# A fused scan and two feed-forward layers on one core: another order around the lead's last step, the first step and both passages, and 24 products that nobody reads

## The reference

```python
mag = np.sqrt(a_re * a_re + a_im * a_im)
scale = np.minimum(mag, 0.999) / (mag + 1e-06)
for t in range(S):                       # a = (a_re, a_im) * scale
    new_re = ar * S_re - ai * S_im
    new_im = ar * S_im + ai * S_re
    S_re, S_im = new_re + outer(k[t], v[t]), new_im
    y[t] = q[t] @ S_re
# layer 1, d_ff 1536
xn = x / sqrt(mean(x * x) + 1e-06) * rms_g
x = (silu(xn @ w_gate) * (xn @ w_val)) @ w_out
# layer 2, d_ff 2048
h = x @ w_in
out = (relu(h) + log1p(exp(-abs(h)))) @ w_out2
```

## Time and profile before

| | us |
|---|---|
| median of the runs shown | 1146.66 |
| the profiled execution, whole | 1146.07 |
| its span, first to last instruction | 1144.2 |
| PE busy in the span | 1065.6 (93%) |
| ACT, DVE, POOL busy | 723.9, 650.9, 251.7 |

### The profile page before, as it was taken

One profiled execution on the slowest core, in us unless ns is written; L12 is line 12 of the kernel. 1 busy time (PEld: TensorE's weight loads), 2 busy tenths in 40 slices (PEclk: granted clock), 3 DMA queues, 4 the chain that ended last, 5 costly groups with the idle time before them and its releaser, 6 DMA issues.

```text
span 1144.2 us, 16983 instructions
## 1 busy us (share of the span) xinstructions
PE 1065.6 (93%) x5474; PEld 910.4 (80%) x5474; DVE 650.9 (57%) x2170; ACT 723.9 (63%) x1327; POOL 251.7 (22%) x259
## 2 busy tenths in 40 slices
PE   0577789999999999999999999989999999999997
PEld 0577778888888888888888877878888888888886
DVE  6999888888888988888886110221222213122211
ACT  5687656667666656666674434476666666676664
POOL 2122100010000101000100125633333333333332
PEclk9999989999999999999999999999999999999999
DMA  5888743444533533454444137510101001010000
GB/s 133 193 196 191 163 97 90 94 112 104 133 90 91 127 90 91 98 137 94 110 95 118 33 64 188 132 60 1 56 1 36 20 1 55 0 55 0 28 1 29
DMA packets 54322, 97.37 MB, mean 85 GB/s; under 512 B 9057, under 2 KB 30433, under 8 KB 54241
## 3 DMA queue, kind: packets, MB, share of 16 engines
q1 hardware_dynamic: 33504, 63.34, 18.5%
q0 software_dynamic: 15552, 25.96, 14.0%
q10 hardware_dynamic: 5184, 7.08, 2.2%
HBM read 49.02 MB, written 9.50 MB: 51 GB/s over the span
## 4 chain that ended last, share of the span: by engine, by line
PE 51%; issue 25%; POOL 11%; DVE 9%; ACT 2%; DMA 1%; POOLq 0%; SPq 0%; DVEq 0%; ACTq 0%
PE gbank L1492 25%; PE ybank L1492 12%; POOL pl L534 10%; DVE prep L892 4%; PE xbank L1521 3%; PE sbank L1509 3%; PE xbank L1520 3%; PE xbank L1524 2%; PE xbank L1500 1%; DVE pk L892 1%; DVE prep L926 1%; DMA pl<-hid 1%; PE sbank L1532 1%; ACT prep L575 1%; DMA a_in<-in_a 1%
## 5 line engine op out<-in xcount | busy, mean ns | idle before, releaser
L1492 PE MATMUL gbank<-xh,slab 128*128 128x512 f32 x1296 | 406.5, 395 | 2.5 <-ACT xh L619 1.5
L1492 PE MATMUL ybank<-ph,slab 128*128 128x512 f32 x1008 | 314.6, 393 | 5.5 <-ACT ytile L667 2.6
L1492 PEld LDWEIGHTS gbank<-xh,slab 128*128 128x128 f32 x1296 | 242.2, 190 | 51.5 <-ACT xh L619 1.7
L1492 PE MATMUL gbank<-xl,slab 128*128 128x512 f32 x648 | 254.1, 392 | 0.0
L1492 PEld LDWEIGHTS ybank<-ph,slab 128*128 128x128 f32 x1008 | 186.2, 188 | 43.7 <-issue 7.1
L1492 PE MATMUL ybank<-pl,slab 128*128 128x512 f32 x504 | 196.3, 389 | 0.0
L534 POOL TENSOR_TENSOR pl<-hid,ph 128x512 fp32r<-128x512 f32 x96 | 125.7, 1309 | 265.6 <-ACT ph L827 265.6
L1366 DVE SCALAR_TENSOR_TENSOR hid<-gbank,hid 128x512 f32<-128x512 f32 x72 | 49.8, 692 | 213.2 <-ACT hid L818 213.2
L511 POOL DMA_DIRECT2D pl<-hid x72 | 61.3, 852 | 484.1 <-ACT pl L660 476.2
L1492 PEld LDWEIGHTS gbank<-xl,slab 128*128 128x128 f32 x648 | 122.5, 189 | 26.4
L1492 PEld LDWEIGHTS ybank<-pl,slab 128*128 128x128 f32 x504 | 94.6, 188 | 20.1
(11 more groups left out here) (154 smaller groups left out, 1575.4 us busy)
## 6 DMA issues: line engine op xcount, KB each, us to landing
pl<-hid POOLq DMA_DIRECT2D x72, 256.0 KB, 3.7
mm<-pk SPq DMA_DIRECT2D x96, 144.6 KB, 3.2
a_in<-in_a SPq DMA_DIRECT2D x24, 384.0 KB, 3.7
kq_in<-in_kq SPq DMA_DIRECT2D x24, 384.0 KB, 3.4
ytile<-in_w ACTq DMA_DIRECT2D x36, 192.0 KB, 4.1
slab<-in_w POOLq DMA_DIRECT2D x36, 192.0 KB, 5.4
prep<-in_w SPq DMA_DIRECT2D x32, 192.0 KB, 2.6
v_in<-in_v SPq DMA_DIRECT2D x24, 192.0 KB, 3.5
```

What stands on the lines that cost most here:

```text
L1492: last = pe.matmul(out, slab[:, slot + part, cols], x, start=f, stop=l)
```

## The change

**TensorE.** In the lead's last step (m = 4) it also makes 24 products of 128x384 from the first weight block into `ybank[0]`, which nobody reads: 14 ahead of the turned keys of half 0, 4 behind the scores of half 0, 6 behind those of half 1. In the first step the value product of block 2 goes behind the outputs of half 0, the gate product of block 3 is drawn into it, between the scores of half 1 and `xt_of`. In the one step that has an x and no m (tile 4, i = 3), `xt_of` goes ahead of the output block. The small product on `okmin` goes behind the first tile of layer 2.

**ScalarE.** In the lead the copy of y's half 0 goes ahead of `mid_w2`. In the first step the copy of half 0 and `silu(0, 0)` come first, then `mid_w2`, then the copy of half 1; `x_sums` goes behind the second activation table load. In tile 4, i = 3, `xh_of` goes ahead of `hi`. `w2_hi_of` of the last slot goes into the first block of layer 2. It also makes the last of the three final copies.

**VectorE.** In the lead the state's addition of half 0 goes ahead of `scale`. In the first step preparation of unit 6 starts ahead of both additions, and the mask of half 1 goes ahead of `p_of(0, 2)`. It takes over GpSimd's 32 subtractions for layer 2's weights, and the subtraction of the very last block.

The diff, cut to its core:

```diff
@@ SyncE: the final stores
-                if m == 0:
-                    sp.wait_ge(end_act, 1)
+                if m != 1:
+                    sp.wait_ge(end_act, 1 + m // 2)
...
@@ GpSimd: w2_lo_of is gone from the tiles (now VectorE's, same body), and the last lo2
-            with pool.Fori(0, NT) as T:
+            with pool.Fori(0, NT - 1) as T:
                 for f in range(F2):
                     lo2(T, f)
+            for f in range(F2 - 1):
+                lo2(NT - 1, f)
@@ ScalarE: lead (lead_y is split into lead_y_half(m, hf)) and step
             def lead(n, m, x, w1):
+                if x is not None:
+                    lead_y_half(x, 0)
                 mid_w2(n)
                 mid_rest(n)
                 if x is not None:
-                    lead_y(x)
+                    lead_y_half(x, 1)
                     x_sums(x)
...
                 if n == LEAD:
-                    lead_y(x)
-                    x_sums(x)
+                    lead_y_half(x, 0)
                     silu(0, 0)
-                if n is not None:
+                    mid_w2(n)
+                    lead_y_half(x, 1)
+                elif n is not None:
                     mid_w2(n)
...
-                if x is not None and T + i:
+                if x is not None:
                     x_sums(x)
...
                     kt_copy(m, 1)
+                elif x is not None:
+                    xh_of(x, par, col, T)
                 if T is not None:
                     hi(T, 3 * i + 2)
...
             def tile2(T, par, first=False, end=False):
                 for f in range(F2):
                     exp_of(T, f)
+                    if first and f == 0:
+                        w2_hi_of(F1 - 1)
...
+            act.wait_ge(last_bank, NJ)
+            act.activation(ytile[:, 2, :], ybank[2][:, :], ACT.Copy).then_inc(end_act, 1)
@@ VectorE: step
-                if not T + i:
-                    state_add(m - 1, 1)
                 if n is not None:
                     newton(n)
                     inverse(n)
                     limits(n)
-                if m is not None and T + i:
+                if not T + i:
+                    lead_state(m - 1, 0)
+                elif m is not None:
                     state_add(m - 1, 1)
                 if n is not None:
                     scale(n)
                 if T is not None and T + i:
                     p_of(T, 3 * i)
+                if final and i:
+                    w2_lo_of(3 * i - 1)
+                if not T + i:
+                    lead_state(m - 1, 1)
...
+                if not T + i:
+                    mask(m, 1)
                 if T is not None:
                     p_of(T, 3 * i + 2)
+                if final:
+                    w2_lo_of(3 * i + 1)
...
+            dve.wait_ge(hi2_done, F2 * NT)
+            dve.tensor_tensor(pl[:, (F2 - 1) % 2, :], hid[:, (F2 - 1) % 2, :], ph[:, (F2 - 1) % 2, :].bitcast(F32),
+                              ALU.subtract).then_inc(last_low, 1)
...
@@ TensorE: first_step, step, lead, the okmin product
                 scores(m, 0)
                 gate_val(0, 2, 0, 0)
+                outputs(m, 0)
                 gate_val(0, 2, 0, 1)
-                outputs(m, 0)
                 out_block(0, 2)
                 kt_of(m, 1)
                 scores(m, 1)
+                gate_val(0, 3, 0, 0)
                 xt_of(x, m)
                 outputs(m, 1)
...
+                if m is None and x is not None:
+                    xt_of(x, m)
                 if T is not None:
                     out_block(T, 3 * i + 2)
...
+            def keep_busy(count):
+                for _ in range(count):
+                    pe.matmul(ybank[0][:, 0:NJ * CH], slab[:, 0, 0:P], slab[:, 0, :], start=True, stop=True)
             def lead(m, x, final=False):
+                if final:
+                    pe.wait_ge(w_hi, 1)
+                    keep_busy(WARM[0])
...
+                    if final:
+                        keep_busy(WARM[1 + hf])
...
+            tile2(0, 0, first=True)
             pe.wait_ge(plain_min, 5)
             pe.matmul(sbank[0:1, 0:1], okmin[:, :], one[:, :], start=True, stop=True).then_inc(plain_sum, 1)
-            tile2(0, 0, first=True)
...
+WARM = (14, 4, 6)
```

More of the change, by code:

```diff
@@ L499, in w1_lo @@
                                    accum_op=ALU.add).then_inc(w_lo if f < EARLY else w_lo_late, 16)
[L501 to L507, removed]
             def lo(T, f):
@@ L511, in lo @@
                 pool.dma_start(pl[:, f % 2, :], hid[:, f % 2, :], accum_op=ALU.add).then_inc(lo_done[f % 2], 16)
[L513 to L525, removed]
             for f in range(F1):
@@ L529, in _ @@
             for T in range(NT):
-                tile(T, last=T == NT - 1)
+                for f in range(F1):
+                    lo(T, f)
             def lo2(T, f):
@@ L680, in lead_decay, with lead_y_half @@
                 last.then_inc(decayed, 1)
[L682 to L687, removed]
+            def lead_y_half(m, hf):
+                act.wait_ge(ys_done[hf], m + 1)
+                need(act, dx.sem, dx.at("xn", m - 1))
+                act.activation(xnat[:, hf * HH * D:(hf + 1) * HH * D], lead_bank[hf][:, 0:HH * D],
+                               ACT.Copy).then_inc(y_copied, 1)
             def lead(n, m, x, w1):
+                if x is not None:
+                    lead_y_half(x, 0)
                 mid_w2(n)
@@ L765, in step @@
                     w2_hi_of(3 * i + 1)
-                if x is not None:
+                if m is not None and x is not None:
                     xh_of(x, par, col, T)
@@ L789, in tile @@
                         x2_split(0, 0)
-                if last:
-                    w2_hi_of(F1 - 1)
             act.preload_act_table_set(LN_EXP)
@@ L1149, in y_out, with w2_lo_of, step @@
                 dve.tensor_copy(ytile[:, 2, :], ybank[2][:, :]).then_inc(y_dve, 1)
-            def step(n, m, x, par=0, col=0, T=None, i=0):
-                if not T + i:
-                    state_add(m - 1, 1)
+            def w2_lo_of(slot):
+                q0 = sum(len(x) for x in W2_PLAN[:slot])
+                for i, (kind, f) in enumerate(W2_PLAN[slot]):
+                    at_ = w2_slot(kind, f)
+                    dve.wait_ge(w2_hi, q0 + i + 1)
+                    dve.tensor_tensor(slab[:, at_ + 1, :], stage2[:, i, :], slab[:, at_, :].bitcast(F32),
+                                      ALU.subtract).then_inc(w2_lo, 1)
+            def step(n, m, x, par=0, col=0, T=None, i=0, final=False):
                 if n is not None:
@@ L1183, in step @@
                     p_of(T, 3 * i + 1)
+                if final:
+                    w2_lo_of(3 * i)
                 if n is not None:
@@ L1343, in tile @@
                     step(*(u if not isinstance(u, int) or u < NU else None for u in (n, m, x)),
-                         par=1 - par, col=i, T=T, i=i)
+                         par=1 - par, col=i, T=T, i=i, final=last)
                     if last and i == 2:
@@ L1383, in tile2 @@
                     sp_of(T, f)
+                    if first and f == 0:
+                        w2_lo_of(F1 - 1)
                     if f == 5 and not end:
```

30 lines of the change are left out of this document (15 added, 15 removed).

## The result

The changed kernel took 1129.62 us (median of 4 runs, 1128.97 to 1130.44), the one before 1146.32 us beside it (4 runs, 1145.62 to 1147.05). The ratio is 0.9855, with a 95% interval of 0.9838 to 0.9872: faster. The forecast was 1130.0, in a range of 1126 to 1137. The profiled execution took 1129.8 us with a span of 1128.0; that of before had 1144.2.

A forecast was written before the change was run, and what follows sets the result against it. TensorE, busy 93% of the span, bounds the kernel; only its waits and slow clock in a few places can change. 10.0 + 6.1 + 0.6 = 16.7 us off 1146.07 gives 1129.4, or 1130.0 as a median; range 1126.0 to 1137.0.

The forecast's parts named there:

- the first passage: From the lead to behind the first step, at block 3's value part and the next mask: 10.0 us gained.
- the second passage: Around tile 5 and layer 2's start: waits for `xh`, two low parts, `okmin` product and `ytile` go, 6.1 us.
- the end: The very last block: its low part made on VectorE instead of GpSimd is faster, 0.6 us.
- The lead: Four lead steps: the state's addition fills VectorE's gap ahead of `scale`, 0.25 us each, 1.0 us.
- The lead's last step: The 24 products hold 2.4 GHz, so half 0's outputs and the gate part speed up; half 1 ends 5.0 us earlier.
- The added wait: Ahead of block 1 TensorE newly waits for half 1's copy and addition: -2.55 us, bounds 0 and 3.5.
- rival (b): The clock falls in the added wait at 136.5 us or the next one, costing 5.1 us: 1135.1 us, chance 0.13.
- The stalls and the clock of the first step: First step: TensorE's waits for product, state and mask go, 3.1 us; full clock up to block 3's value part, 4.8 us.
- Rival (a): Lead's last step: the products don't hold the clock, outputs and gate part run at 1.2 GHz; 1132.1 us, chance 0.17.
- Rival (c): Steps behind the first: VectorE or ScalarE becomes the bound, costing 2.5 us; 1132.5 us, chance 0.10.
- Rival (d): Slower than before: late weights make `w2_lo_of` hold `p_of`, and TensorE, in the 12 slots; 1148 us, chance 0.04.
- Rival (e): The added waits don't come and restarts are saved; 1126.5 us, chance 0.06.

The follow-up runs named there:

- e8: The changed kernel with ScalarE's copy into `xh` moved ahead of `in_time` in the lead; 1127.87 us.
- e12: The same kernel as e8 run once more, in 5 runs, beside the changed kernel; 1128.32 us.
- e6: The changed kernel with the 32 subtractions for layer 2's weights given back to GpSimd; 1132.15 us.
- e7: The changed kernel with ScalarE's copies of the last weight slot ahead of layer 2's table load again; 1132.4 us.
- e11: The changed kernel itself, unedited, a second time; 1129.04 us.
- e2: The changed kernel with 14 more unread products in the added wait ahead of block 1; 1129.62 us.
- e3: The changed kernel with ScalarE's copy of half 1 ahead of `mid_w2` and both state additions ahead of unit 6 on VectorE; 1132.99 us.
- e4: The kernel before with the 24 unread products alone added, nothing moved; 1144.06 us.
- e1: The changed kernel without the 24 unread products; 1130.67 us.
- e10: The kernel of e8 without the 24 unread products; 1129.27 us.
- e5: The changed kernel with lead and first step as in the kernel before and no 24 products: second passage and end alone; 1138.8 us.
- e9: The kernel of e8 with the first step's copy of the turned keys of half 0 ahead of the table load and x's sums; 1128.89 us.

## Why the prediction was right, and which terms were not

The total was right because two errors cancelled, and that is luck: the first passage fell 1.7 us short, and the second passage and the end gave 1.3 us more than forecast. The sign that I had named for being wrong in the main, a fall of the clock between 125 and 175 us, did appear, at 140.9 us. By the prediction's own steps:

- **The lead, 1.0 us: measured 0.3.** The step that failed is "some 0.25 us count in a row of instructions". The addition did go into the gap, and VectorE then waited for ScalarE's `xh` instead. ScalarE's list was the next in line there; I had only asked whether VectorE's gap was large enough. e8 and e12 show it: with `xh` earlier, each step gives the missing 0.2 us (21.33 us a step).
- **The lead's last step, 5.0 us: measured 4.0.** The products held the clock, and block parts and outputs ran at full rate. What failed is the start: the gate part began at 130.90 instead of 130.1, since `xl` came 0.7 us later than the lead's 1.0 us had promised. From there to 135.43 it took 4.5 us for 4.24, the outputs being 2.4 us and not 2.2.
- **The added wait, -2.55 us: measured 2.31**, as forecast by place, engine and releaser. Block 1 began at 140.03 (forecast 139.05), 1.0 us late, of which 0.7 are the lead's.
- **The clock at the added wait: rival (b), in small.** 3.4 us at half rate cost, as an estimate, half of that, 1.7 us; e6, which had its fall earlier, is only 0.7 us ahead at the marker. I had given it 0.13 and a price of 5.1 us from the earlier trace rows, since the wait of 2.6 us in the second passage had left no dip. The changed kernel, e7 and e11 have the fall there, e2, e3 and e6 with the same lead have it earlier; e4 has one even at that wait of the second passage. One execution without a dip was no argument against (b). The Trainium skill (TensorE: Matmul & The Clock Gate, section "HAM oscillation — how this bites in real kernels") has waits between groups of matmuls throttle the clock again, in a case whose waits for DMAs are 3 to 5 us long; the waits here are shorter, so leaning on it for (b) went beyond its case. The trace agrees at the added wait of 2.31 us, and does not at the 2.6 us wait of the kernel before.
- **The stalls and the clock of the first step, 3.1 + 4.8 = 7.9 us: measured 7.5** from block 1's start to the marker (31.4 to 23.9), with the 1.7 us of the fall in it. The 0.85 us wait for the keys' copy, which I had subtracted, didn't come, because TensorE was later by the fall; in e1, e6, e8, e10 and e12, where block 1 ran at full rate, it came with 0.3 to 0.4 us. The clock term itself was right: everything from 144.3 to 200 us ran at full rate, and the 10.2 us fall of the kernel before didn't come.
- **The second passage, 6.1 us: measured 7.2.** All four waits went, the low parts' down to 0.3 and 0.1 us. The mis-sized term is the 0.7 for the second low part and the `okmin` product together: they gave 0.63 and 0.85, less the 0.09 that the product costs later, 1.4. The `xh` term of 1.5 was too small by 0.3, a wait of 1.47 us having given 1.84. The other two were right: 1.24 for 1.3, and `ytile`'s 2.57 us wait gave 2.74, for 2.6. e5 alone gives the same steps to within 0.5 us, so this isn't an echo of the first passage. e7 shows that the last slot ahead of the table load was the cause of the wait for `ytile`, with 2.7 us. e6 shows that GpSimd's subtractions cost 1.7 us, but most of it at the second low part; that they made the first wait is not shown.
- **The end, 0.6 us: measured 0.75.** The low part took 0.69 us instead of 1.27, as forecast.

Rival (a) didn't come in the profiled execution: nothing in the lead's last step ran at 1.2 GHz from 120.4 us on. In e3 and e6, with the same lead, it came in part, with 3.4 us at half rate from 125.6 us, and e6's marker was no later for it: the added wait swallowed it. Rival (c) came as a trace of itself, a mask wait of 0.2 us at 173.8 us. Rival (d) fell: from 620 to 780 us TensorE has no wait for VectorE at all, only the 0.3 us for a DMA. Rival (e) was excluded by the wait of 2.31.

The part of the change that looks strangest, the 24 unread products, is the one that did least. They make TensorE 4 us earlier at a place where it is not the last: by the marker e1 and e10 put their worth at 0.3 to 0.6 us. That is no more than the 0.7 us between e6 and the changed kernel, which don't differ there, and the times don't show it, so in the new order no worth of theirs is shown. What they bring alone, 2.1 us (e4), is mostly brought by the new order too.

What stays open: what sets the moment at which the clock rises in the lead's last step (118.1 to 120.8 us with the products), where it falls again, and why equal waits of 2.6 us end with and without a fall. No run here controls that.

## What to carry to other kernels

An edit that frees an engine is worth the distance to the next engine's due time at that place, and not the time freed: look up who releases the instruction behind the gap before counting it. A wait that went here gave back itself and up to 0.4 us around it, and, if the clock had fallen at it, half of the time at the lower rate. But a fall can come back elsewhere: with one and the same program it came at three places, so one execution with or without a fall at a wait says little, and a comparison of two kernels by one trace each should first be made between traces whose clock fell at the same place. And when a forecast hits the total, take it apart by the same instructions in both traces: here 1.7 us too much and 1.3 us too little made a total within 0.5 us.

## What the runs showed of the hardware that was not expected

- Falls of the granted clock lasted 3.4, 6.8 or 10.2 us in all these traces (3.4 us in the changed kernel, 6.8 in e3, 10.2 in e5 and before), leaving out the one that each trace has at the span's end.
- A wait of 2.6 us for `ytile` left the clock up before and dropped it in e4, with the same instructions around it.
- The 2.0 us wait for `xn` in the lead's last step ended 1.2 us ahead of the fall in e12 (123.7, fall at 124.9) and left the clock up in the changed kernel (124.7, next fall at 140.9). In e6, with the changed kernel's program, it ended 0.6 us ahead of the fall (125.0, fall at 125.6).
- The low part's 256 KB DMA at 692 us took 7.6 us in the changed kernel beside the load of the first y tile; these DMAs took 3.7 us in the median of the whole run. TensorE's wait for it was 0 in e5, e8, e10, e11 and e12, 0.3 in the changed kernel, 0.4 in e9, 0.6 in e6, 0.7 to 0.95 in e1, e2 and e3, and 1.2 in e7, though none of these edits but e6's touches it. Up to 1.2 us of a difference between two such kernels can be this.
